# An expert's first 128 rows worked before the routing is finished, experts in alternating order, and logits of four late tiles by column groups

## The reference, cut to what matters

```python
kv  = einsum('bhsd,bhse->bhde', k, v);  a = einsum('bhsd,bhde->bhse', q, kv)
x   = (a / rms(a) * g_norm)              # 4 x 8 heads of 64 -> 2304 x 512
p   = probs / (probs.sum(-1) + 1e-9)     # dense mixture, 4 experts, all tokens
x1  = sum_e p[:, e] * (relu(x @ w1[e]) @ w2[e])            # 512 -> 1024 -> 512
lg  = norm(x1) @ norm(expert_emb).T / tau                  # 8 experts
idx = argmax(lg);  gate = softmax(lg)[idx]                 # one expert per token
out[tokens of e] = gate * (relu(x1 @ w1b[e]) @ w2b[e])     # routed mixture
```

## Time and profile before

| | |
|---|---|
| runs | 1142.08, 1143.15, 1145.65 us |
| profiled execution | 1145.34 us; first to last instruction (span) 1143.8 us |
| mean granted TensorE clock | 0.994 |
| PE busy | 1119.3 us (98%), 6210 matmul records |
| VectorE / ScalarE / POOL busy | 728.7 / 456.9 / 655.3 us |
| last dense matmul ends | 840.4 us |
| first routed matmul starts | 857.9 us |
| last routed matmul ends | 1134.3 us |

### The profile page before, as it was taken

One profiled execution on the slowest core, in us unless ns is written; L12 is line 12 of the kernel. 1 busy time (PEld: TensorE's weight loads), 2 busy tenths in 40 slices (PEclk: granted clock), 3 DMA queues, 4 the chain that ended last, 5 costly groups with the idle time before them and its releaser, 6 DMA issues.

```text
span 1143.8 us, 18712 instructions
## 1 busy us (share of the span) xinstructions
PE 1119.3 (98%) x6210; PEld 985.1 (86%) x6211; DVE 728.7 (64%) x1160; ACT 456.9 (40%) x812; POOL 655.3 (57%) x609
## 2 busy tenths in 40 slices
PE   8999999999999999999999999999989999999996
PEld 8888899998899888999898888999887888888885
DVE  4867888888866788888866788888662222222221
ACT  4783444444434534444434534444222222222220
POOL 2597776899868777799868777777330111111101
PEclk9999999999999999999999999999989999999998
DMA  9945777877612448877612438877469759337960
GB/s 256 271 140 182 267 265 273 285 274 259 228 37 90 139 137 300 293 276 261 217 44 86 155 115 312 284 276 257 155 238 391 265 189 381 140 111 296 360 252 13
DMA packets 102433, 250.87 MB, mean 219 GB/s; under 512 B 8254, under 2 KB 48190, under 8 KB 94171
## 3 DMA queue, kind: packets, MB, share of 16 engines
q1 hardware_dynamic: 97360, 235.18, 59.5%
q0 software_dynamic: 4800, 14.72, 3.5%
q10 hardware_dynamic: 203, 0.05, 0.0%
HBM read 170.99 MB, written 79.98 MB: 219 GB/s over the span
## 4 chain that ended last, share of the span: by engine, by line
PE 90%; DVE 6%; ACT 1%; issue 1%; POOL 0%; DMA 0%; SPq 0%; DVEq 0%; POOLq 0%; ACTq 0%
PE ps L1289 28%; PE ps L1291 27%; PE ps L1290 27%; PE ps L1499 2%; PE ps L1247 1%; DVE x_rows L976 1%; PE ps L1465 1%; DVE hT_lo L958 1%; PE ps L1217 1%; PE ps L1367 1%; DVE attn_rows L897 1%; PE ps L1230 1%; DVE hT_lo L965 1%; PE ps L1258 1%; DVE ahead_lo L984 0%
## 5 line engine op out<-in xcount | busy, mean ns | idle before, releaser
L1289 PE MATMUL ps<-w_hi,hT_hi 128*128 128x512 f32 x576 | 227.0, 394 | 2.1 <-DVE x_rows L976 2.0
L1289 PE MATMUL ps<-x_ops_hi,w_hi 128*128 128x384 f32 x672 | 226.8, 338 | 1.9 <-DVE sum L946 1.9
L1291 PE MATMUL ps<-x_ops_hi,w_lo 128*128 128x384 f32 x672 | 225.8, 336 | 0.0
L1291 PE MATMUL ps<-w_hi,hT_lo 128*128 128x512 f32 x576 | 225.2, 391 | 0.0
L1290 PE MATMUL ps<-w_lo,hT_hi 128*128 128x512 f32 x576 | 225.0, 391 | 0.0
L1290 PE MATMUL ps<-x_ops_lo,w_hi 128*128 128x384 f32 x672 | 224.9, 335 | 0.0
L976 DVE SCALAR_TENSOR_TENSOR x_rows<-ps,dense_probs,x_rows 128x512 f32<-128x512 f32 x270 | 190.2, 739 | 16.9 <-PE ps L1291 16.8
L615 POOL DMA_INDIRECT out_dram<-y_rows,row_ids x22 | 22.6, 1028 | 236.0 <-DVE y_rows L1180 141.5
L495 POOL TENSOR_TENSOR w_lo<-w_raw,w_hi 128x512 fp32r<-128x512 f32 x96 | 146.3, 1543 | 12.3 <-ACT w_hi L709 8.0
L1170 DVE TENSOR_TENSOR rhT_lo<-ps,rhT_hi 128x512 fp32r<-128x512 f32 x44 | 28.4, 687 | 172.0 <-ACT rhT_hi L835 172.0
L1289 PEld LDWEIGHTS ps<-x_ops_hi,w_hi 128*128 128x128 f32 x672 | 126.2, 188 | 6.4 <-DVE sum L946 3.2
(11 more groups left out here) (204 smaller groups left out, 1996.8 us busy)
## 6 DMA issues: line engine op xcount, KB each, us to landing
w_slots<-split_parts SPq DMA_DIRECT2D x64, 1024.0 KB, 5.8
w_raw<-in_moe_w_dram SPq DMA_DIRECT2D x96, 512.0 KB, 3.6
ahead_raw<-in_moe_w_dram SPq DMA_DIRECT2D x64, 512.0 KB, 7.0
split_parts<-ahead_hi SPq DMA_DIRECT2D x64, 512.0 KB
split_parts<-ahead_lo SPq DMA_DIRECT2D x64, 512.0 KB
row_tile<-dispatched_rows POOLq DMA_DIRECT2D x20, 257.0 KB, 5.7
kv<-in_k_dram SPq DMA_DIRECT2D x16, 288.0 KB, 6.8
kv<-in_v_dram SPq DMA_DIRECT2D x16, 288.0 KB, 7.7
```

The lines of the kernel that those rows point to most:

```text
L1289: mm(out_, ah, bh, start=(first and m == 0), stop=False, skip_group_check=not final or not first)
L1291: last = mm(out_, al, bh, start=False, stop=(final and m == n - 1), skip_group_check=not final or not first)
```

## The change

Seen in the diff: (1) In dense step 46 VectorE ranks the experts by the rows counted in the first twelve tiles (`order_places`, five parts, one after each of five `add`s). The places then go to the largest, the smallest, the second largest, the second smallest expert and so on. (2) The first 128 rows of the largest become tile 0, the early one. SP loads them during step 46 and 47, TensorE transposes them in the tail (`flip_rows(0, 0)` after the second `down`), and its 24 up and 24 down matmuls and 8 hidden transposes are put between the routing of the last block and the tables, in place of the identity matmuls. Its second-half `w2` pieces are loaded when the last dense `down` is done, its first half before. (3) The logits of tiles 12 to 15 are made by column groups and one transpose back per block, like those of the first four blocks. (4) The tables are worked out with the places permuted and counted without the early rows; two remainders of the early tile's hidden rows (`rt_half`) lie among them on VectorE. (5) The routed loop begins with tile 2; tile 1's work is written out ahead of it.

```diff
+    STAR_AT = 46
+    T0 = TT - TPT
...
-            sp.wait_ge(up_done, OPS * STEPS)
+            sp.wait_ge(star_ready, 2)
+            e_star = sp.value_load(tab_s[0:1, 0:1], min_val=0, max_val=E2 - 1)
+            e_next = sp.value_load(tab_s[0:1, 1:2], min_val=0, max_val=E2 - 1)
+            r_star = sp.value_load(tab_s[0:1, 2:3], min_val=P, max_val=E2 * CAP)
             for s in range(2):
                 sp.wait_ge(s_out[s], 32 * (NAHEAD // 2))
-            for n in range(2 * PCS):
-                load_first(n)
+            sp.wait_ge(scattered, 16 * T0)
+            sp.dma_start(xs[:, 0, :], rows[bass.ds(r_star, P), :]).then_inc(first_rows_in[0], 16)
+            sp.wait_ge(up_done, OPS * STEPS)
+            for c in range(2):
+                load_piece(c, e_star, 0, c)
+            for c in range(2):
+                load_early(PCS + 2 + c, c)
+            for c in range(2):
+                sp.wait_ge(part_in[0][c], 16)
+                load_piece(2 + c, e_star, 0, 2 + c)
+            for c in range(2):
+                sp.wait_ge(part_in[0][c], 32)
+                load_piece(PCS + c, e_next, 0, c)
...
+            for c in range(2, PCS):
+                load_early(2 * PCS + c, c)
             sp.wait_ge(tab_ready, 1)
             first_rows = [sp.value_load(tab_r[0:1, s:s + 1], min_val=0, max_val=E2 * CAP + P) for s in range(2)]
-            sp.wait_ge(scattered, 16 * TT)
-            for s in range(2):
-                sp.dma_start(xs[:, s, :], rows[bass.ds(first_rows[s], P), :]).then_inc(first_rows_in[s], 16)
-            for s in range(2):
-                sp.wait_ge(first_rows_in[s], 16)
-            for n in range(2 * PCS, 4 * PCS):
-                load_first(n)
+            sp.wait_ge(scattered, 16 * T0)
+            sp.wait_ge(scattered_late, 16 * TPT)
+            sp.dma_start(xs[:, 1, :], rows[bass.ds(first_rows[0], P), :]).then_inc(first_rows_in[1], 16)
+            sp.dma_start(xs[:, 0, :], rows[bass.ds(first_rows[1], P), :]).then_inc(first_rows_in[2], 16)
+            for c in range(2):
+                for half in range(2):
+                    n = (2 * PCS + c) * PIECE + half * PIECE // 2
+                    m = (PCS + c) * PIECE + half * PIECE // 2
+                    sp.dma_start(W[:, n:n + PIECE // 2].bitcast(F32), parts[e_star, :, m:m + PIECE // 2]).then_inc(part_in[1][c], 16)
+            sp.wait_ge(ry_done, 2)
+            for c in range(2, PCS):
+                sp.wait_ge(part_in[0][c % 2], 48)
+                load_piece(PCS + c, e_next, 0, c)
+            for c in range(PCS):
+                sp.wait_ge(part_in[1][c % 2], 32 + c // 2 * 16)
+                load_piece(3 * PCS + c, e_next, 1, c)
...
+            pool.wait_ge(rx_done, 2)
+            pool.wait_ge(gi_copied, 2)
+            load_rows(3, 1)
...
+            for s in range(2):
+                store(s, s)
+                pool.wait_ge(rx_done, s + 3)
+                pool.wait_ge(gi_copied, s + 3)
+                load_rows(s + 4, s)
+            with pool.Fori(1, PAIRS) as i:
...
+            def copy_by_tile(b):
+                m = (BLOCKS[b][1] - BLOCKS[b][0]) * EW
+                act.wait_ge(lgt_done, b + 1)
+                A(lgt[0:m, :], ps[0:m, 3, 0:P], ACT.Copy).then_inc(lgt_copied, 1)
...
+            for s in range(2):
+                act.wait_ge(s_out[s], 32 * (NAHEAD // 2))
+            rx(0, 0)
+            for t in range(T0, TT):
                 route(t)
                 if t == TT - 4:
                     exponentials(NB - 3)
+                if t in (T0 + 1, T0 + 3):
+                    copy_by_tile(block_of(t))
             exponentials(NB - 2)
             exponentials(NB - 1)
+            for half in range(2):
+                relu_half(0, half)
+                rt_half(0, 0, half)
             act.wait_ge(tab_ready, 2)
             tiles = act.value_load(tab_n[0:1, 0:1], min_val=TT, max_val=KT)
-            rx(0, 0)
             rx(1, 1)
-            relu_rows(0)
-            rt_parts(0, 0)
-            with act.Fori(0, PAIRS) as i:
+            rx(2, 0)
+            relu_rows(1)
+            rt_parts(1, 1)
+            rx(3, 1)
+            relu_rows(2)
+            rt_parts(2, 0)
...
+            def order_places(part):
+                if part == 0:
+                    dve.wait_ge(rank_read, NB - 3)
+                    step(V.tensor_tensor(ec(0), run[:, :], ebase[:, :], ALU.subtract))
+                    step(V.scalar_tensor_tensor(ec(1), ec(0), float(E2), iota_e[:, :], ALU.mult, ALU.subtract))
+                    step(V.tensor_tensor(cmpo[:, :, :], ec(1).unsqueeze(1).to_broadcast(oe), ec(1).unsqueeze(2).to_broadcast(oe), ALU.is_gt))
+                if part == 1:
+                    step(V.tensor_reduce(ec(0), cmpo[:, :, :], AX.X, ALU.add))
+                    step(V.tensor_scalar(ec(1), ec(0), -2.0, float(2 * E2 - 1), ALU.mult, ALU.add))
+                    step(V.scalar_tensor_tensor(ec(1), ec(0), 2.0, ec(1), ALU.mult, ALU.min))
+                    step(V.tensor_tensor(chosen_at[:, :, :], ec(1).unsqueeze(1).to_broadcast(oe), knum[:, 0:E2].unsqueeze(2).to_broadcast(oe), ALU.is_equal))
...
+                        if k == STAR_AT and j < 5:
+                            order_places(j)
...
+                if n == 2:
+                    rx(0, 0)
+                    V.tensor_copy(early_gi[:, :], xs[:, 0, D:D + 2]).then_inc(gi_copied, 1)
+                if n == 8:
                     read_logits(NB - 3)
                     choose(NB - 3)
                 if n == 9:
                     read_ranks(NB - 3)
                     place(NB - 3)
                     gates(NB - 3)
-                if n == 10:
-                    read_logits(NB - 2)
+            read_logits(NB - 2)
...
+            step(V.tensor_tensor(cmpo[:, :, :], chosen_at[:, :, :], ec(0).unsqueeze(1).to_broadcast(oe), ALU.mult))
+            step(V.tensor_reduce(ec(0), cmpo[:, :, :], AX.X, ALU.add))
...
+            rt_half(0, 0, 0)
...
+            step(V.scalar_tensor_tensor(ec(3), ec(1), 0.0, two[:, :], ALU.is_gt, ALU.max))
+            step(V.tensor_tensor_scan(ec(4), unit[:, :], ec(3), 0.0, ALU.mult, ALU.add))
...
+            rt_half(0, 0, 1)
...
+                if t == T0:
+                    pe.wait_ge(rx_split, 1)
...
+            def early_up(half, chunks):
+                pe.wait_ge(rx_split, 1)
+                pe.wait_ge(y_used, TPT * STEPS)
+                if half:
+                    pe.wait_ge(lg_read, NB)
+                for c in chunks:
+                    for d in range(2):
+                        pe.wait_ge(part_in[0][d], 16 * (c // (KC // 2) + 1))
+                    cs = slice(c * P, (c + 1) * P)
+                    m = c // (KC // 2) * 2 * PIECE + c % (KC // 2) * F + half * 512
+                    last = three(ps[:, 1 + half, :], [(rxh[:, 0, cs], rxl[:, 0, cs], W[:, m:m + 512], W[:, PIECE + m:PIECE + m + 512])], c == 0, c == KC - 1)
+                if chunks[-1] == KC - 1:
+                    last.then_inc(rh_done, 1)
+            def flip_half(n, half):
+                pe.wait_ge(rh_relu, 2 * n + half + 1)
+                for c in range(4):
+                    m = half * 512 + c * P
+                    last = tr(ps[:, 3 + half, c * P:(c + 1) * P], hs[:, m:m + P], ident[:, :])
+                last.then_inc(rt_done, 1)
+            def early_down(chunks):
+                half = chunks[0] // (FCH // 2)
+                pe.wait_ge(rt_split, half + 1)
+                pe.wait_ge(early_in[half], 32)
+                for c in chunks:
+                    cs = slice(c * P, (c + 1) * P)
+                    m = (2 * PCS + 2 if half else PCS + 2) * PIECE + c % (FCH // 2) * D
+                    last = three(ps[:, 5, :], [(rhh[:, 0, cs], rhl[:, 0, cs], W[:, m:m + D], W[:, PIECE + m:PIECE + m + D])], c == 0, c == FCH - 1)
+                if chunks[-1] == FCH - 1:
+                    last.then_inc(ry_done, 1)
             for n, (kk, j) in enumerate(TAIL):
                 down(kk, j)
+                if n == 1:
+                    pe.wait_ge(h_lo, 4 * LAST + 1)
+                    flip_rows(0, 0)
+                if n in (7, 11):
+                    logits_by_token(NB - 3 + n // 11, LAST)
                 if n in (3, 5, 7, 9, 11):
                     flip(T0 + n // 2 - 1, LAST)
-                if n in (4, 6, 8, 10):
-                    logits(T0 + n // 2 - 2, LAST)
+                if n in (6, 10):
+                    logits_by_tile(NB - 3 + n // 10, LAST)
                 if n == 9:
                     ranks(NB - 3, LAST)
             flip(TT - 1, LAST)
             logits(TT - 2, LAST)
             ranks(NB - 2, LAST)
             logits(TT - 1, LAST)
+            early_up(0, (0, 1))
             ranks(NB - 1, LAST)
+            early_up(0, (2, 3))
+            early_up(1, (0, 1))
+            pe.wait_ge(rank_read, NB)
+            flip_half(0, 0)
+            early_up(1, (2, 3))
+            early_down((0, 1))
+            flip_half(0, 1)
+            early_down((2, 3))
```

(25 more changed lines are left out.)

203 lines of the change are left out of this document (118 added, 85 removed).

## The result

The changed kernel took 1133.41 us (median of 4 runs, 1133.18 to 1134.49), the kernel before, beside it, 1144.4 (4 runs, 1142.08 to 1145.65): a ratio of 0.9908, 95% interval [0.9888, 0.9928]. A second timing with more runs gave 1135.5 (5 runs, 1133.71 to 1135.94) against 1143.53 (15 runs): 0.9924 [0.9911, 0.9938]. It is faster by 8 to 11 us; 1132.2 had been predicted. The profiled execution took 1133.41 us, its span is 1131.8 (before 1143.8).

A forecast was written before the change was run, and what follows sets the result against it. TensorE bounds the kernel (90% of the wait chain), lacking useful work for about 14.2 us before the routed stage. One tile's -12.50, +1.1, +0.2 and 0.2 for straight code gave -11.0: 1132.2 us from 1143.15, range 1129.0 to 1138.0.

The forecast's parts named there:

- One tile, -12.50: Routed stage: one of 22 tiles leaves the stretch after 857.9 us, saving 12.50 us.
- Step 46, +0.2: Dense step 46: `order_places` adds 18 small VectorE operations, 3.5 us uncovered, taken as costing 0.2 (0 to 0.6).
- The early rows in the tail, 0.44 + 0.3: Tail: four transposes of early rows cost 0.44 us, a possible wait of `flip(12)` for VectorE's remainder 0.3.
- The logits, 1.1 saved less 0.2: Tail: column groups for two blocks save 1.1 us of TensorE; reading logits after the last `add` comes 0.2 later.
- Tables and `rt_half`: Tables: extra steps and a remainder among them put `tab_r` at 851.8 us instead of 851.12, VectorE not waiting.
- Tile 1's first `up`, +1.1: Loop's start: tile 1's first `up` at 859.0 us, where tile 0's was at 857.92; bounds 857.6 to 862.
- The straight code, 0.2: Ahead of the routed loop: longer straight code costs 0.2 us.
- Rival 1: Under the early tile the clock falls to 0.50, tile 1 starts at 861.4, gain 8.6, 1134.6 us; chance 0.25.
- Rivals 2, 3: 2: chain ahead of tables grows, 1135 to 1139.7 us, chance 0.10; 3: early weights or rows late, 1143, chance 0.05.
- Rival 4: Routed places of one tile: weights late, two stalls of 7.8 us, together 15.6, giving 1147.8 us; chance 0.08.
- The sum: Whole kernel: -12.50 + 1.1 + 0.2 = -11.2, less 0.2 for straight code: -11.0 us.

The follow-up runs named there:

- early_late: The changed kernel with the early tile's matmuls and remainders put behind the tables instead of beside them: 1147.34 us, ratio 1.0040 to the kernel before.
- early_only: The changed kernel with the logits of tiles 12 to 15 made tile by tile as before: 1134.17 us, ratio 0.9922 to the kernel before.
- logits_only: The kernel before with only the logits of tiles 12 to 15 by column groups, no early tile: 1145.14 us, ratio 1.0011.
- loads_moved: The changed kernel with VectorE's value load after tile 1's remainder and POOL reading tile 3's row number before its wait: 1134.09 us, ratio 0.9908 to before.
- ones_in_row: The changed kernel with the largest expert first, then from the smallest up (5, 1, 1, 2, 2, 2, 3, 5 tiles): 1150.34 us, ratio 1.0053 to before.
- early_bank: The changed kernel with another result bank for the early up, its first group ahead of the last transposes: 1133.35 us, ratio 0.9911 to the kernel before.

## Why the prediction was right, and which of its terms were not

- **One tile, -12.50:** right. First to last result is 12.5 shorter, the window of 13.00 is as full as before, and `early_late` shows that the tile is gained by overlap.
- **Step 46, +0.2:** nothing. The interval between the `product`s of steps 46 and 47 is 15.52 after, 15.53 before.
- **The early rows in the tail, 0.44 + 0.3:** right. `early_only` has 29.07 + 6.45 = 35.52 to the tables, before 34.80: 0.72.
- **The logits, 1.1 saved less 0.2:** this step failed. Measured is +0.33 (`logits_only`: 28.06 + 7.07 = 35.13). I had put two tiles at 0.85 between 0.67 and 1.01, by the number of tiles. But the 16 records of two tiles last as long as the 24 of three (1.00 and 1.01 to the next matmul), so the tiles in a column group run beside each other, and the upper bound was the price of the records. And I had read the prices from the group's own start: from the matmul before it to the second one after it, two tiles cost 1.19, and three cost 1.19 too in the kernel before (615.24 to 616.89, less 0.47), where one by token costs 0.89. So two tiles save 0.59 and not 0.77. The rest of the forecast saving went in waits that I had put at nothing: 0.17 for ScalarE's copy ahead of the second group, 0.44 at the ranks of tiles 12 and 13, and the read of the logits behind the last `add` brings the tables 0.54 later and not 0.2. The prediction had weighed the rule of the Trainium skill (TensorEngine Tiling (Array Packing), Key Properties) that changing the mode drains TensorE, and had let 0.3 hang on it. Around a group without a wait the rows leave room for 0.09 ahead of its first record and 0.10 behind it, which may be such a drain; the rows do not show that it is. With it the tables started 1.1 later than before (35.94 against 34.80), where 0.2 sooner was forecast.
- **Tables and `rt_half`:** close. 4.82 where the clock held, 4.9 forecast; 5.27 and 5.53 where it fell, for then VectorE does wait 0.49 for the copy, against "it doesn't wait". The last table and tile 1's rows came in the order that was told, and the transposes came 2.75 behind the load's issue, as the 2.7 of the earlier trace rows.
- **Tile 1's first `up`, +1.1:** mis-sized, +2.7. Of the 1.6 more, 1.35 lie ahead of the tables (1.2 of it the logits), 0.35 in the tables, -0.3 in a sooner issue and 0.2 to 0.3 behind the rows. There VectorE's value load, of which the prediction said nothing but its place, stands in the path: moving it gave 0.5 (`loads_moved`).
- **The straight code, 0.2:** not seen. At the loop's entry TensorE stands 0.38 us (at 867.02), before it stood 0.51 there (at 866.34).
- **The opening, not foreseen, +0.6 to +1.4:** tile 3's rows are asked for by POOL only when tile 1's gates are read, and arrive 6.8 us later (859.23 to 865.98) beside SP's 1 MB pieces, while rows alone took 2.7. The prediction had told what is queued behind tile 1's load, not what tile 3's is queued behind.
- **Rival 1, the clock:** its mechanism came in the gap in four of the five executions with the changed kernel's order there: 0.50 from 842.3 to 845.7 in the first (844.1 to 847.5 in the second). The thin stretch was followed by real matmuls at 841.75, and that didn't prevent it. By the Trainium skill (TensorE: Matmul & The Clock Gate, What's actually happening) activity releases the throttle: the rows agree with that for the way back, which came at 845.7 and not at 850.7 as with the earlier trace rows. So the fall was half as long, and cost 0.5 to 0.7, not 2.4 (861.4 less 859.0). The two executions without that fall, `ones_in_row` and `early_only`, had theirs in the opening, behind a wait of 1.49 and 1.34 us for tile 3's rows: 0.50 from 868.8 to 872.3 and from 867.2 to 870.6. There it cost 1.5: their openings are 23.6 and 23.5, against 22.2 in the second execution of the changed kernel (wait 1.52) and 22.0 in `early_bank` (wait 1.28). So each of the six executions with the early tile in the gap and the thin stretch whole had one fall, and with one group of matmuls moved into that stretch (`early_bank` and the three with it) there was none, in the gap or in the opening, in four. Six and four executions don't show how surely that group holds the clock.
- **Rivals 2, 3:** didn't come; no remainder in the changed kernel waits more than 0.49 for its copy within the tables, and no `up` or `down` of the early tile waits for weights. **Rival 4:** didn't come, and `ones_in_row` shows that it depends on the order: 13.2 us, 9.75 of them waiting and most of the rest the clock's fall, against the 15.6 priced.
- **The sum:** -12.5 + 2.7 + 0.6 to 1.4 is -8.4 to -9.2 for the change itself, 2 less than the -11.0 forecast, and the longer timing says -8.0 to -8.7. That the first timing gave -11.0 is probably in part chance: in its traces 2.7 us of the difference lie ahead of the mark. The case and the range were right; the match of the numbers was better than the working.

## What to carry to other kernels

Where TensorE has to wait for a table, real work that needs no table is worth most of its length (8 to 9 of 12.5 us here), even where the clock falls under part of it, as long as its weights and rows are there first. Compare two executions from the last mark that both share, not from time zero, or chance in the untouched part is taken for effect. And price a small group of another shape from the start of what comes before it to the second start of what comes after it, take out what it waits for, and don't scale it by the number of groups that run side by side.

## What the runs showed of the hardware that I had not expected

- A VectorE remainder with two SBUF inputs took 0.65 us in most steps and 4.36 and 3.30 us in two of one execution, POOL busy beside it in both cases; the one with a PSUM input stayed at 0.56 in all 48 steps.
- The granted clock fell to 0.50 with TensorE busy 3.00 of 3.00 us in the records, after 3.35 us of transposes and 8-column matmuls (838.40 to 841.75), and it fell within a wait of 7.12 us for weights (945.6 to 952.7), at 950.8, and came back at 957.6, 4.9 us after the matmuls did.
- Logits in column groups take 1.00 us for two tiles (16 records) and 1.01 for three (24); amid dense matmuls, where nothing waits, both cost TensorE 1.19.
- A load of one tile's rows took 2.7 us from issue to landing alone, and 6.8 us beside the pieces of weights (859.23 to 865.98; 7.5 in `loads_moved`, 859.92 to 867.41).
